# The second mixture of a two-mixture kernel on one core: counting of bids in groups of four tiles, search steps at finer points, a list chain on 43-wide arrays

## The chip, the cores and the metric

The program runs on one core of a Trainium2 chip. Its time is device microseconds of that core. It was timed in three runs (1503.53 to 1504.03 us, median 1503.86 us). Shares, chains and single durations come from one further execution with the profiler, which took 1500.03 us and whose span is 1498.2 us.

## The reference

An attention-like stage gives x (4608 tokens by 512). A first mixture of eight experts follows (top expert by a softmax router), then a second one, and this change is about the second:

```python
def _moe2_ref(x, w_gate, w1, w2):
    N, D = x.shape                       # 4608, 512
    E = w_gate.shape[1]                  # 8
    cap = N // E                         # 576
    flat = (x @ w_gate).flatten()
    order = np.argsort(-flat)
    assigned = -np.ones(N, dtype=np.int64)
    counts = np.zeros(E, dtype=np.int64)
    for idx in order:                    # best (token, expert) pair first
        tok, e = (int(idx) // E, int(idx) % E)
        if assigned[tok] >= 0 or counts[e] >= cap:
            continue
        assigned[tok] = e
        counts[e] += 1
    for e in range(E):
        mask = assigned == e
        h = np.maximum(x[mask] @ w1[e], 0.0)
        out[mask] = h @ w2[e]            # w1 512x1024, w2 1024x512
```

So every expert takes exactly 576 tokens, and which ones depends on the order in which experts fill up.

## The kernel before, in words

Three stages follow each other. Up to about 250 us runs the attention-like stage. Then come T1 = 43 tiles of 128 sorted rows through the first mixture ("stage one" below); after each tile VectorE computes the eight router scores of its rows from y (`scores`, L1198 to L1205). The rest is the second mixture: eight **phases**, one for each expert in the order in which the experts fill, each of T2 = 5 tiles of rows.

A tile is 48 **products** on TensorE (128x128 stationary, 512 columns, in fp32r). Every operand is split into a high and a low part, so each layer takes three passes (high by high, high by low weights, low by high weights): 12 products for each half of the first layer and 24 for the second. Beside them stand 4 transposes of the next tile's rows (L723) and 8 of h (L730). ScalarE makes the high parts and the copies, VectorE the low parts: `rows_low` (xT_lo, L1183), `hT_low` (hT_lo, L1189, two instructions a tile) and `weights_low` (w_lo, L1237, eight pieces of 1024 columns a phase). Weights come by SP's queue: eight pieces of 512 KB a phase, issued once the expert is known, with at most two on their way, and ScalarE waits until all eight have landed (L473, L936).

Which expert fills next, and with which rows, is found by **select** (L1263 to L1383) on VectorE with small steps on TensorE (`search`, L766 to L789). The scores are an array of 128 partitions x 43 tiles x 8 experts.

- *bids*: each row bids for its best open expert (`best`, `bid`, L1285 to L1292).
- *eight rounds* of a search for the threshold at which the first expert is full, 15 thresholds each: `cmp` on VectorE (128x645), a *count* on TensorE, `ind` on VectorE, a *spread* over partitions on TensorE, then `tn`, `n_i`, `low_i`, `thr_i`, which give the next 15 thresholds. The count is one matmul for each of the 43 tiles, with 128 bid columns as stationary side (8 of them in use) and 15 columns moving, plus one for the room left: 44 matmuls.
- *the list chain*: sums above and at the threshold, the expert (L1336, releases the weight load), ties, then the row numbers of the expert's rows: `ohb` (128x5504), `oha2`, `ra2`, one list step of 43 matmuls on TensorE (L787), `gat_i` and `sca_i` (L1376, releases the gathers of POOL), and last the scores of the filled expert and of the taken rows are masked (L1379 to L1383).

Each step is a pair: VectorE raises one semaphore (`ask`, L1275) and waits for TensorE's answer. Nineteen steps make a select. Of the order: a table gives each step a **point** among the products of the running phase. TensorE reaches a point, waits there for VectorE, does the step and goes on with the products; all its instructions stand in one order. The table of before has eight points a tile, and the next expert's select runs beside the running phase; its first eight steps (four rounds) run a phase earlier, from tile 3 on. VectorE puts its own duties for the products (`rows_low`, `hT_low`, `weights_low`) right behind its request of a step, before it waits for the answer (`beside_step`, L1250). Select 0, and the first four rounds of select 1, have no products beside them. VectorE runs selects 2 to 7 in a hardware loop of two selects an iteration.

Of the kernel before, what the change touches and what calls it, by code (L numbers as in the profile page):

```python
# [30 lines left out]
P = 128  # L31
# [28 lines left out]
def build(nc, q, k, v, g_norm, w_gate, w_og, w1, w2, w_gate2, w21, w22, out, debug=None):  # L60
# [4 lines left out]
    PT = 96  # L65
# [19 lines left out]
    STEPS = 2 * R + 3  # L85
    EARLY = 8
    gaps = [0] + [1, 2] * R + [4, 7]
    at, where = 0, []
    for n in range(STEPS):
        at += gaps[n]  # L90
        where.append(at)
    cycle = 8 * T2
    POINTS = sorted((x - where[EARLY]) % cycle for x in where)
    assert len(set(POINTS)) == STEPS and POINTS[0] == 0

    DUTIES = {n: [] for n in range(STEPS)}
    for g in range(T2):
        for kind, due, need in (("h", 8 * g, 8 * g + 5), ("x", 8 * g + 4, 8 * g + 8)):  # L100
            p = min([x for x in POINTS if x >= due], default=cycle)
            assert p <= need
            DUTIES[(POINTS.index(p) + EARLY) % STEPS if p < cycle else EARLY].append((kind, g))
    assert all(n != EARLY or ("x", T2 - 1) not in d for n, d in DUTIES.items())


    LOW_BESIDE = [EARLY - 4, EARLY - 3, EARLY - 2, EARLY - 1, EARLY + 4, EARLY + 5, EARLY + 6, EARLY + 7]
    PIECES = len(LOW_BESIDE)

    with ExitStack() as ctx:  # L110
# [24 lines left out]
        ones_h = sb("ones_h", [P, P], F16)  # L135
        before = sb("before", [P, P])
# [4 lines left out]
        segment = sb("segment", [PT, E, G1])  # L141
# [16 lines left out]
        onehot = sb("onehot", [PT, E, G1])  # L158
# [51 lines left out]
        s_wp = [sem(f"piece_loaded{i}") for i in range(2)]  # L210
# [5 lines left out]
        s_clear = sem("bids_cleared")  # L216
# [17 lines left out]
        s_sc = sem("scores_done")  # L234
        s_sel = sem("select_dve")
# [97 lines left out]
        bid = sb("bid", [P, T1, P], F16)  # L333
# [3 lines left out]
        cmp = sb("cmp", [P, T1, NTH], F16)  # L337
        a3 = sb("a3", [P, T1, E])
        b3 = sb("b3", [P, T1, E])
        taken = sb("taken", [P, T1, E])  # L340
        room_n = sb("room_n", [P, P], F16)
        ind = sb("ind", [P, NTH], F16)
        best = sb("best", [P, T1])
        m43 = sb("m43", [P, 4, T1])
        tn = sb("tn", [P, NTH])
        n_i = sb("n_i", [P, R], I32)
# [55 lines left out]
        def _(sp):  # L402
# [56 lines left out]
            def load_phase(kk, u):  # L459
# [27 lines left out]
        def _(pool):  # L487
# [84 lines left out]
            pool.memset(bid[:, :, :], 0.0).then_inc(s_clear, 1)  # L572
# [29 lines left out]
        def _(pe):  # L602
# [73 lines left out]
            def in_parts(ps, acts, w, cols, chunks, low_w, low_x, done, point):  # L676
# [3 lines left out]
                per = chunks * 3 // (2 if chunks == KC else 4)  # L680
                for i in range(3 * chunks):
# [9 lines left out]
                    if i % per == per - 1:  # L691
                        point(i // per)
# [71 lines left out]

            cps, aps = sel_ps

            def search(kk, n):
# [3 lines left out]
                if n < 2 * R and n % 2 == 0:  # L771
# [4 lines left out]
                elif n < 2 * R:  # L776

                    mm = pe.matmul(aps[:, 0:NTH], ones_h[:, :], ind[:, :], start=True, stop=True)
                elif n == 2 * R:

                    pe.matmul(cps[:, 0:2 * E], ones_h[:, :], sums_h[:, :, :], start=True, stop=True)
                    mm = pe.matmul(aps[:, 0:E], before_h[:, :], sums_h[:, 1, :], start=True, stop=True)
                elif n == 2 * R + 1:
# [8 lines left out]
            def searches(kk, i):  # L792


                if i in POINTS:
                    n = POINTS.index(i) + EARLY
                    ahead = kk + 1 if n < STEPS else kk + 2
                    if not (isinstance(kk, int) and ahead >= E):
                        search(ahead, n % STEPS)
# [631 lines left out]
```

## Time and profile before

| | us |
|---|---|
| median of three runs | 1503.86 |
| profiled execution | 1500.03 |
| its span | 1498.2 |
| last y of stage one made (ScalarE, L906) | 793.4 |
| first product of the second mixture (TensorE, L687) | 877.3 |
| TensorE busy in 787 to 890 us | 37.7 of 103 |
| TensorE busy in 890 to 1498 us | 580.8 of 608 |
| VectorE busy in 890 to 1498 us | 382.5 of 608 |

A row of the timeline gives start, duration, engine, line, instruction, and in brackets how long the engine was idle before it and who released it. "PE" is TensorE, "DVE" VectorE, "ACT" ScalarE, "POOL" GpSimd. Matmul ends are modelled, so the cost of a group on TensorE is best read as the distance from its start to the next start.

### The profile page before, as it was taken

Reading aid. Unit: us, or ns where it says so; the run is one execution under the profiler, and the core shown is the slowest. Engines: PE = TensorE matmul, PEld = TensorE weight load, DVE = VectorE, ACT = ScalarE, POOL = GpSimd, SP = SyncE. Lnnn points to the kernel's source line nnn. Section 1 sums busy time; section 2 is a strip of 40 time slices with the busy share of each in tenths; the row PEclk is TensorE's granted clock in tenths of the full one; section 3 lists DMA queues with packets and bytes.
Section 4 is the critical chain, followed back from the end, with each engine's and each line's share of the span. In section 5 each row is a group of like instructions: output and inputs, shape, how many; then the busy total and the mean of one; then the engine's idle time right before and its main releaser. Section 6 shows DMA issues by size and latency. Waiting matters only on the chain.

```text
span 1498.2 us, 26945 instructions
## 1 busy us (share of the span) xinstructions
PE 1315.6 (88%) x9724; PEld 1084.6 (72%) x9724; DVE 974.1 (65%) x2214; ACT 441.3 (29%) x784; POOL 397.5 (27%) x324
## 2 busy tenths in 40 slices
PE   5988718898999999999993169999999999999997
PEld 5877616786888888888882157878777777787885
DVE  1566793677567677776667768585758585767420
ACT  1655522122222222222220032423232323233431
POOL 1244426747616172480000001111111111111110
PEclk9989858999999999999996569999999999999999
DMA  9999128694514143241100304040404132222310
GB/s 218 253 271 289 57 45 297 220 352 154 156 43 155 42 157 106 89 146 49 43 22 15 124 18 148 30 152 30 145 30 132 50 117 65 82 93 84 104 32 18
DMA packets 71168, 173.48 MB, mean 116 GB/s; under 512 B 11624, under 2 KB 30136, under 8 KB 70400
## 3 DMA queue, kind: packets, MB, share of 16 engines
q1 hardware_dynamic: 46576, 108.61, 24.8%
q0 software_dynamic: 12368, 40.92, 8.6%
q10 hardware_dynamic: 12096, 22.19, 4.7%
q8 instruction: 87, 1.43, 0.4%
q14 instruction: 41, 0.34, 0.1%
HBM read 130.47 MB, written 41.23 MB: 115 GB/s over the span
## 4 chain that ended last, share of the span: by engine, by line
PE 67%; DVE 16%; DMA 6%; issue 5%; POOL 5%; ACT 1%; SPq 0%; DVEq 0%; POOLq 0%; ACTq 0%
PE bank L687 50%; PE bank L775 5%; PE bank L730 4%; POOL w_lo L524 3%; PE o_ps L648 2%; DMA xst<-x_rows,tok_i 2%; DMA x_sorted<-xst 1%; DMA v_sb<-in_v 1%; PE kv_ps L614 1%; POOL w_hi L522 1%; DMA w_sb<-in_moe_w 1%; PE bank L723 1%; PE bank L716 1%; DVE xrow L1052 1%; PE qt_ps L636 1%
## 5 line engine op out<-in xcount | busy, mean ns | idle before, releaser
L1202 DVE SCALAR_TENSOR_TENSOR bank<-bank,factor,wg2b 128x512 f32<-128x512 f32 x344 | 260.6, 758 | 10.8
L1189 DVE TENSOR_TENSOR hT_lo<-bank,hT_hi 128x512 fp32r<-128x512 f32 x166 | 107.0, 685 | 194.0 <-ACT hT_hi L932 185.0
L899 ACT ACTIVATE h<-bank 128x512 f32<-128x512 f32 x166 | 99.2, 598 | 356.8 <-PE bank L687 335.7
L687 PE MATMUL bank<-w_hi,xT_hi 128*128 (+1 forms) x664 | 193.1, 413 | 10.7 <-POOL w_lo L524 6.4
L687 PE MATMUL bank<-w_lo,xT_hi 128*128 (+1 forms) x664 | 190.6, 403 | 0.4 <-DVE w_lo L1237 0.4
L687 PE MATMUL bank<-w_hi,hT_hi 128*128 (+1 forms) x664 | 180.8, 411 | 6.2 <-DVE score L1205 3.3
L687 PE MATMUL bank<-w_hi,xT_lo 128*128 (+1 forms) x664 | 182.9, 397 | 0.0
L578 POOL DMA_INDIRECT xg<-y_rows,gat_i x40 | 41.6, 1040 | 502.3 <-DVE sca_i L1376 283.1
L687 PE MATMUL bank<-w_lo,hT_hi 128*128 (+1 forms) x664 | 173.4, 402 | 0.0
L687 PE MATMUL bank<-w_hi,hT_lo 128*128 (+1 forms) x664 | 171.0, 398 | 0.0
L687 PEld LDWEIGHTS bank<-w_hi,xT_lo 128*128 128x128 f32 x664 | 125.6, 189 | 30.5 <-issue 0.2
L687 PEld LDWEIGHTS bank<-w_lo,hT_hi 128*128 128x128 f32 x664 | 125.9, 191 | 29.4
L687 PEld LDWEIGHTS bank<-w_hi,hT_lo 128*128 128x128 f32 x664 | 124.2, 189 | 29.1
L687 PEld LDWEIGHTS bank<-w_hi,xT_hi 128*128 128x128 f32 x664 | 120.1, 193 | 33.8 <-issue 12.4
L687 PEld LDWEIGHTS bank<-w_lo,xT_hi 128*128 128x128 f32 x664 | 123.9, 191 | 28.0 <-DVE w_lo L1237 0.9
L687 PEld LDWEIGHTS bank<-w_hi,hT_hi 128*128 128x128 f32 x664 | 119.1, 191 | 28.2 <-issue 6.2
L524 POOL TENSOR_TENSOR w_lo<-w_sb,w_hi 128x1024 fp32r<-128x1024 f32 x56 | 134.3, 2398 | 4.5
L522 POOL CAST w_hi<-w_sb 128x1024 fp32r<-128x1024 f32 x56 | 58.3, 1041 | 183.0 <-DMA w_sb<-in_moe_w 183.0
L585 POOL DMA_INDIRECT out<-y,sca_i x40 | 44.8, 1120 | 230.2 <-ACT y L927 228.1
L1183 DVE TENSOR_TENSOR xT_lo<-bank,xT_hi 128x512 fp32r<-128x512 f32 x83 | 57.2, 690 | 72.6 <-ACT xT_hi L917 71.3
L932 ACT ACTIVATE hT_hi<-bank 128x512 fp32r<-128x512 f32 x166 | 90.8, 598 | 45.6 <-PE bank L730 33.7
L906 ACT ACTIVATE y<-bank,factor 128x512 f32<-128x512 f32 x43 | 29.5, 687 | 218.4 <-PE bank L687 193.5
(238 smaller groups left out, 1803.1 us busy)
## 6 DMA issues: line engine op xcount, KB each, us to landing
w_sb<-in_moe_w SPq DMA_DIRECT2D x112, 512.0 KB, 5.0
y_rows<-y ACTq DMA_DIRECT2D x43, 256.0 KB
x_sorted<-xst SPq DMA_DIRECT2D x41, 260.0 KB
xg<-x_sorted ACTq DMA_DIRECT2D x41, 260.0 KB
k_sb<-in_k SPq DMA_DIRECT2D x16, 576.0 KB, 15.5
v_sb<-in_v SPq DMA_DIRECT2D x16, 576.0 KB, 17.3
q_sb<-in_q SPq DMA_DIRECT2D x8, 1152.0 KB, 20.6
x_rows<-xrow POOLq DMA_DIRECT2D x16, 576.0 KB, 6.3
```

Source lines behind the costliest of these rows:

```text
L522: pool.tensor_copy(w_hi[:, 1 - e % 2, cols(i)], w_sb[:, e % 2, cols(i)]).then_inc(s_phi, 1)
L524: pool.tensor_tensor(w_lo[:, e % 2, cols(i)], w_sb[:, e % 2, cols(i)], w_hi[:, 1 - e % 2, cols(i)].bitcast(F32), ALU.subtract).then_inc(s_ ...
L578: pool.indirect_dma_start(out=xgs[w % 2][:, 0:DM], out_offset=None, in_=y_rows[:, :], in_offset=bass.IndirectOffsetOnAxis(ap=gat_i[:, w:w ...
L585: pool.indirect_dma_start(out=out[:, :], out_offset=bass.IndirectOffsetOnAxis(ap=sca_i[0:rows, w:w + 1], axis=0), in_=ys[w % 2][0:rows, :] ...
L687: mm = pe.matmul(ps, a[:, i % chunks, :], b[:, i % chunks, cols], start=(i == 0), stop=(i == 3 * chunks - 1))
L730: mm = pe.transpose(th_ps[half][:, i * P:(i + 1) * P], h[:, half * 4 + i:F:FC], ident[:, :])
L775: mm = pe.matmul(cps[:, 0:NTH], bid[:, g, :], cmp[:, g, :], start=False, stop=(g == T1 - 1))
L899: act.activation(h[:, half * HALF:(half + 1) * HALF], h_ps[half][:, :], ACT.Relu).then_inc(s_h, 1)
L932: act.activation(hT_hi[:, half * 4:(half + 1) * 4, :].rearrange("p a b -> p (a b)"), th_ps[half][:, :], ACT.Copy).then_inc(s_hT, 1)
L1183: dve.tensor_tensor(xT_lo[:, :, :].rearrange("p a b -> p (a b)"), tx_ps[:, :], xT_hi[:, :, :].rearrange("p a b -> p (a b)").bitcast(F32), ...
L1189: dve.tensor_tensor(hT_lo[:, half * 4:(half + 1) * 4, :].rearrange("p a b -> p (a b)"), th_ps[half][:, :], hT_hi[:, half * 4:(half + 1) * ...
L1202: ch.link(dve.scalar_tensor_tensor(out=prod_ps[:, :], in0=y1_ps[t % 2][:, :], scalar=factor[:, t:t + 1], in1=wg2b[:, e, :], op0=ALU.mult, ...
```

## The change

1. **Dense count.** `bid` shrinks from 43x128 to 43x8 columns. Four tiles go into one matmul: 32 stationary columns (4 tiles x 8 experts) and 60 moving ones (4 tiles x 15 thresholds). Eleven matmuls replace 43; the wanted numbers are the four diagonal blocks. A new step copies the 32x60 result to SBUF (`dense`, VectorE), and five small matmuls add the blocks and the room (TensorE). A round has three steps where it had two.
2. **List chain on 43-wide arrays.** Each row's bid is kept as one number (`code`), each row's owner too (`owner`), and ties and ranks are worked out on 128x43 arrays in place of 128x43x8 ones. Sums use the dense count; a step for ties is new. `ohb` is made in two halves with a duty between them.
3. **Points.** A point stands behind every second product: 24 a tile. The 29 steps of a select are laid out with ten points a round; it starts 13 points ahead of a phase, so five steps (one round and two steps of the next) run a phase earlier. A point of tile 4 holds the list step, and ten points on stands the first count of the select after it. The first phase has a table of its own, seven points a round, and select 1 runs wholly inside it.
4. **Duties.** The low parts of the next phase's first two weight pieces and of the last tile's h stand behind the list, ahead of the masking.
5. **Weights.** All eight pieces are issued at once, each with a semaphore of its own; ScalarE waits for a piece, not for all.
6. **Between the stages.** The last tile's router scores come from TensorE (4 transposes, a copy, 4 matmuls) in place of eight products on VectorE; the bids and first comparison of 40 of the 43 tiles are made two tiles earlier; the low parts of the first phase's first four pieces stand behind select 0's list.

Core of the diff:

```diff
+    GROUP = 4
+    SUMS, TOTALS, TIES, RANKS, LIST = range(3 * R, 3 * R + 5)
+    PER_TILE = 24
+    def timed(start, per_round, behind):
+        at = [start + per_round * r + 2 * i for r in range(R) for i in range(3)]
+        for gap in behind:
+            at.append(at[-1] + gap)
+        at += [at[LIST] - 8, at[LIST] + 3]
+        return at
+    WHERE = timed(-13, 10, (4, 3, 6, 5, 18))
+    FIRST = timed(13, 7, (3, 3, 5, 4, 17))
+        for kind, due, need in (("h", PER_TILE * g + 3, PER_TILE * g + 16), ("x", PER_TILE * g + 13, PER_TILE * g + 24)):
+    LOW_BESIDE = {AFTER_LIST: (0, 1), 1: (2,), 2: (3,), 7: (4,), 8: (5,), 10: (6,), 11: (7,)}
+    FIRST_LOW_BESIDE = {1: (4,), 2: (5,), 4: (6,), 5: (7,)}
...
-                    wait_pos(sp, s_wp[i % 2], (kk * (PIECES // 2) + i // 2) * 16)
                     sp.dma_start(w_sb[:, u, i * w_piece:(i + 1) * w_piece],
-                                 ).then_inc(s_wp[i % 2], 16)
+                                 ).then_inc(s_wp[i], 16)
...
+            pe.wait_ge(s_y, T1)
+            for c in range(KC):
+                mm = pe.transpose(tx_ps[:, c * P:(c + 1) * P], ys[(T1 - 1) % 2][:, c * P:(c + 1) * P], ident[:, :])
+            for c in range(KC):
+                mm = pe.matmul(th_ps[0][:, 0:E], h[:, c * P:(c + 1) * P], wg2_sb[:, c, :], start=(c == 0), stop=(c == KC - 1))
...
-                    pe.matmul(cps[:, 0:NTH], room_n[:, :], ones_h[:, 0:NTH], start=True, stop=False)
-                    for g in range(T1):
-                        mm = pe.matmul(cps[:, 0:NTH], bid[:, g, :], cmp[:, g, :], start=False, stop=(g == T1 - 1))
+                    for g in range(0, T1, GROUP):
+                        some = min(GROUP, T1 - g)
+                        mm = pe.matmul(dps[0:some * E, 0:some * NTH], bid[:, g:g + some, :].rearrange("p g e -> p (g e)"),
+                                       cmp[:, g:g + some, :].rearrange("p g n -> p (g n)"), start=(g == 0), stop=(g + GROUP >= T1))
+                    pe.matmul(cps[0:E, 0:NTH], room_n[:, :], ones_h[0:1, 0:NTH], start=True, stop=False)
+                    for g in range(GROUP):
+                        mm = pe.matmul(cps[0:E, 0:NTH], ident_h[:, g * E:(g + 1) * E], dense[:, g * NTH:(g + 1) * NTH],
+                                       start=False, stop=(g == GROUP - 1))
...
-                    if i % per == per - 1:
-                        point(i // per)
+                    if i % 2 == 1:
+                        point(i // 2)
...
-                act.wait_ge(s_wl, (kk + 2) * 32)
                 for i in pieces:
+                    act.wait_ge(s_wp[i], (kk + 1) * 16)
...
+                if n == AFTER_LIST:
+                    for i in LOW_BESIDE[n]:
+                        weights_low(kk, u, i)
...
+                    ask(dve.tensor_copy(dense[:, :], dps[0:GROUP * E, :]))
-                link(dve.tensor_tensor(b3[:, :, :], b3[:, :, :], over_g(es), ALU.mult))
-                link(dve.tensor_reduce(m43[:, 0, :], b3[:, :, :], AX, ALU.add))
-                link(dve.tensor_tensor(b3[:, :, :], b3[:, :, :], over_e(m43[:, 1, :]), ALU.mult))
-                link(dve.tensor_tensor(a3[:, :, :], a3[:, :, :], b3[:, :, :], ALU.add))
-                link(dve.tensor_tensor(taken[:, :, :], taken[:, :, :], a3[:, :, :], ALU.add))
+                link(dve.scalar_tensor_tensor(out=tied, in0=rank, scalar=spare, in1=tied, op0=ALU.is_le, op1=ALU.mult))
+                link(dve.tensor_tensor(chosen, gteq[:, :, 0], tied, ALU.add))
+                    link(dve.tensor_tensor(tied, chosen, code[:, :], ALU.mult))
+                    link(dve.tensor_tensor(owner[:, :], owner[:, :], tied, ALU.add))
+                link(dve.tensor_scalar(mine, owner[:, :], expert, None, ALU.is_equal))
...
+                    if gs.start == 0:
+                        beside_step(kk, u, HALF_LIST)
...
+                beside_step(kk, u, AFTER_LIST)
```

The order on TensorE between the list step of one select (matmuls bank<-ra,ohb) and the first count of the next (bank<-cmp,bid), inside the loop over phases. Before:

```order
L787 MATMUL bank<-ra,ohb 128x20 x42
...
L730 MATMUL bank<-ident,h 128x128 x3
...
L687 MATMUL bank<-w_hi,xT_lo 128x512 x3
L721 ISA
L723 MATMUL bank<-ident,xg 128x128 [waits y_rows_gathered0]
L723 MATMUL bank<-ident,xg 128x128 x3
L687 MATMUL bank<-w_hi,hT_hi 128x512 [waits y_ready,hT_copied]
L687 MATMUL bank<-w_hi,hT_hi 128x512 x5
L770 ISA
L773 MATMUL bank<-ones_h,room_n 128x15 [waits select_dve]
L775 MATMUL bank<-cmp,bid 128x15 x43
```

Now:

```order
L838 MATMUL bank<-ra,ohb 128x20 x42
L710 MATMUL bank<-w_lo,xT_hi 128x512 x4
L710 MATMUL bank<-w_hi,xT_lo 128x512 [waits xT_low]
L710 MATMUL bank<-w_hi,xT_lo 128x512 x3
L710 MATMUL bank<-w_hi,xT_hi 128x512 x4
L710 MATMUL bank<-w_lo,xT_hi 128x512 x4
L710 MATMUL bank<-w_hi,xT_lo 128x512 [waits xT_low]
L710 MATMUL bank<-w_hi,xT_lo 128x512 x3
L804 ISA
L811 MATMUL bank<-cmp,bid 32x60 [waits select_dve]
L811 MATMUL bank<-cmp,bid 32x60 x9
L811 MATMUL bank<-cmp,bid 24x45
```

Before, 30 products, 12 transposes stood between the two (8 of h, all 24 products of the first layer, 4 transposes of rows, 6 products of the second layer); now 20 products and no transpose.

The order on VectorE from the list's last instruction (sca_i) to the first comparison of the next select. Before:

```order
L1376 SCALAR_TENSOR_TENSOR sca_i<-lst 128x5
L1379 TENSOR_REDUCE m<-a 128x43
L49 REGISTER_ALU
L1380 TENSOR_SCALAR m<-m 128x43 [waits dve_chain]
L1381 TENSOR_SCALAR e<-e 128x8
...
L1299 TENSOR_TENSOR cmp<-best,thr 128x645 [waits dve_chain]
L1188 ISA
L1189 TENSOR_TENSOR hT_lo<-bank,hT_hi 128x512 [waits hT_copied]
```

Now:

```order
L1463 SCALAR_TENSOR_TENSOR sca_i<-lst 128x5
L1319 ISA
L1321 TENSOR_TENSOR w_lo<-w_sb,w_hi 128x1024 [waits weights_high]
L1319 REGISTER_ALU
L1321 TENSOR_TENSOR w_lo<-w_sb,w_hi 128x1024 [waits weights_high]
L1245 ISA
L1246 TENSOR_TENSOR hT_lo<-bank,hT_hi 128x512 [waits hT_copied]
L1245 REGISTER_ALU
L1246 TENSOR_TENSOR hT_lo<-bank,hT_hi 128x512 [waits hT_copied]
L1467 SCALAR_TENSOR_TENSOR room<-e 128x8
L1468 TENSOR_SCALAR m<-m 128x43
```

Two pieces of w_lo and one tile's hT_lo now stand between the list and the masking; the chain from masking to comparison is otherwise the same, without one reduction.

The order on TensorE in tile 0 of the first phase, behind its 24 first-layer products (there is no second layer of an earlier tile yet). Now:

```order
L746 MATMUL bank<-ident,xg 128x128 x3
L811 MATMUL bank<-cmp,bid 32x60 [waits select_dve]
L811 MATMUL bank<-cmp,bid 32x60 x9
L811 MATMUL bank<-cmp,bid 24x45
L815 MATMUL bank<-ones_h,room_n 8x15 [waits select_dve]
L817 MATMUL bank<-dense,ident_h 8x15 x4
L821 MATMUL bank<-ind,ones_h 128x15 [waits select_dve]
L811 MATMUL bank<-cmp,bid 32x60 [waits select_dve]
L811 MATMUL bank<-cmp,bid 32x60 x9
L811 MATMUL bank<-cmp,bid 24x45
L815 MATMUL bank<-ones_h,room_n 8x15 [waits select_dve]
L817 MATMUL bank<-dense,ident_h 8x15 x4
```

Five steps of select 1 stand there in a row with no product between them.

## Rows read from the trace of the kernel before

**Rows 1.** Windows: span, us, busy (count) PE PEld DVE ACT POOL, PEclk, DMA share, GB/s

```profile
890.00:1498.00 608.00, 580.76 (x4940) 469.05 (x4940) 382.48 (x872) 183.15 (x292) 82.25 (x76) 0.99 0.26 81
```

**Rows 2.** Timeline (start, us, engine, line, instruction, shape, count), TensorE, two tiles without steps

```profile
1405.71 1.05 PE L730 MATMUL bank<-ident,h 128*128 128x128 f32 x8
...
1416.40 2.03 PE L687 MATMUL bank<-w_hi,hT_lo 128*128 128x512 f32 x8
1418.27 1.05 PE L730 MATMUL bank<-ident,h 128*128 128x128 f32 x8
```

**Rows 3.** Timeline, TensorE, a count and a spread between products

```profile
1192.20 0.18 PE L773 MATMUL bank<-ones_h,room_n 128*128 128x15 f16 x1
...
1193.33 0.71 PE L687 MATMUL bank<-w_lo,xT_hi 128*128 128x512 f32 x2
...
1194.81 0.18 PE L778 MATMUL bank<-ind,ones_h 128*128 128x15 f16 x1
...
1195.86 1.09 PE L687 MATMUL bank<-w_lo,xT_hi 128*128 128x512 f32 x4
```

**Rows 4.** Timeline, TensorE, the transposes of h that close tiles

```profile
893.23 1.95 PE L730 MATMUL bank<-ident,h 128*128 128x128 f32 x8
...
954.60 1.05 PE L730 MATMUL bank<-ident,h 128*128 128x128 f32 x8
...
1031.52 1.05 PE L730 MATMUL bank<-ident,h 128*128 128x128 f32 x8
```

**Rows 5.** Timeline, from the list step to the next select's first count

```profile
999.88 1.24 PE L787 MATMUL bank<-ra,ohb 128*128 128x20 f16 x43
...
1006.92 0.83 DVE L1299 TENSOR_TENSOR cmp<-best,thr 128x645 f16<-128x645 f32 x1
...
1242.28 0.16 DVE L1285 TENSOR_SCALAR room_n<-room 1x8 f16<-1x8 f32 x1 [3.37 <-issue]
...
1246.31 0.18 PE L773 MATMUL bank<-ones_h,room_n 128*128 128x15 f16 x1 [1.57 <-DVE cmp L1299]
```

**Rows 6.** Groups by shape (count, busy us, mean ns, idle and releaser), VectorE, phases

```profile
L1237 DVE TENSOR_TENSOR w_lo<-w_sb,w_hi 128x1024 fp32r<-128x1024 f32 x59 | 71.5, 1219 | 0.0
L1189 DVE TENSOR_TENSOR hT_lo<-bank,hT_hi 128x512 fp32r<-128x512 f32 x80 | 51.5, 684 | 45.8 <-ACT hT_hi L932 45.6 <-DVE score L1383 0.2
...
L1379 DVE TENSOR_REDUCE m<-a 128x43 f32<-128x344 f32 x7 | 3.5, 504 | 0.0
```

**Rows 7.** Windows around two stops of TensorE, columns as in rows 1

```profile
886.00:898.00 12.00, 8.16 (x116) 7.17 (x114) 8.33 (x18) 4.17 (x6) 0.95 (x1) 0.72 0.08 23
1090.00:1098.00 8.00, 8.00 (x73) 6.27 (x72) 2.32 (x10) 1.15 (x2) 0.99 (x1) 0.79 0.00 0
```

**Rows 8.** Timeline, from the last y to the first phase; then DMA issues

```profile
793.44 0.69 ACT L906 ACTIVATE y<-bank,factor 128x512 f32<-128x512 f32 x1 [6.05 <-PE bank L687]
...
807.58 0.20 PE L773 MATMUL bank<-ones_h,room_n 128*128 128x15 f16 x1 [14.18 <-DVE cmp L1299]
...
839.58 0.14 DVE L1336 TENSOR_SCALAR expert_i<-sc 1x1 int32<-1x1 f32 x1
...
856.06 0.17 DVE L1376 SCALAR_TENSOR_TENSOR sca_i<-lst 128x5 int32<-128x5 f32 x1
...
861.19 5.79 ACT L939 ACTIVATE w_hi<-w_sb 128x1024 fp32r<-128x1024 f32 x6 [67.06 <-SPq L473]
...
877.28 2.05 PE L687 MATMUL bank<-w_hi,xT_hi 128*128 128x512 f32 x4 [0.78 <-ACT xT_hi L917]
...
891.57 0.20 PE L773 MATMUL bank<-ones_h,room_n 128*128 128x15 f16 x1 [3.57 <-DVE cmp L1299]
...
xg<-y_rows,gat_i POOLq DMA_INDIRECT x40, 3.4
```

**Rows 9.** Timeline, TensorE's rank step and VectorE's last part of a list

```profile
1224.64 0.18 PE L784 MATMUL bank<-mtot_h,before_h 128*128 128x1 f16 x1 [1.00 <-DVE mtot_h L1356]
...
1233.22 1.05 DVE L1369 TENSOR_TENSOR ra<-oha,payload 128x860 f16<-128x860 f16 x1
```

More of the change, by code:

```diff
@@ L82, in build @@
     STAGED = 8
[L85 to L98, printed above, removed]
-    for g in range(T2):
[L100 to L103, printed above, removed]
@@ new lines, in build @@
+    WHERE = timed(-13, 10, (4, 3, 6, 5, 18))
+    FIRST = timed(13, 7, (3, 3, 5, 4, 17))
+    EARLY = sum(x < 0 for x in WHERE)
+    POINTS = {x % cycle: n for n, x in enumerate(WHERE[:STEPS])}
+    FIRST_POINTS = {x: n for n, x in enumerate(FIRST[:STEPS])}
+    assert len(POINTS) == STEPS and len(FIRST_POINTS) == STEPS and AFTER_LIST == len(WHERE) - 1
+    assert max(FIRST) < WHERE[0] + cycle
+    DUTIES = {n: [] for n in range(len(WHERE))}
+    FIRST_DUTIES = {n: [] for n in range(len(WHERE))}
@@ L336, in build @@
         ohb = sb("ohb", [P, T1, P], F16)
[L337 to L344, printed above, removed]
-        tn = sb("tn", [P, NTH])
+        sb("rest_of_router", [P, 560])
+        oha2 = sb("oha2", [P, T1, T2], F16)
+        ra2 = sb("ra2", [P, T1, T2, 4], F16)
+        tn = sb("tn", [P, NTH])
+        gteq = sb("gteq", [P, T1, 2], F16)
+        blocks = sb("blocks", [GROUP * E, GROUP, 2])
+        sums = sb("sums", [GROUP * E, 2])
+        spread = sb("spread", [GROUP * E, 2, E], F16)
+        e8 = sb("e8", [P, 4, E])
         n_i = sb("n_i", [P, R], I32)
@@ L770, in search @@
                 pe.wait_ge(s_sel, kk * STEPS + (n + 1))
-                if n < 2 * R and n % 2 == 0:
-                    pe.matmul(cps[:, 0:NTH], room_n[:, :], ones_h[:, 0:NTH], start=True, stop=False)
-                    for g in range(T1):
-                        mm = pe.matmul(cps[:, 0:NTH], bid[:, g, :], cmp[:, g, :], start=False, stop=(g == T1 - 1))
[L776 to L783, printed above, removed]
+                if not isinstance(kk, int):
+                    alone(pe)
@@ L792, in searches @@
             def searches(kk, i):
+                first = isinstance(kk, int) and kk == 0
+                if first and i in FIRST_POINTS:
+                    search(1, FIRST_POINTS[i])
                 if i in POINTS:
[L796 to L799, printed above, removed]
+                    n = POINTS[i]
+                    ahead = kk + 1 if n >= EARLY else kk + 2
+                    if not (first and n >= EARLY) and not (isinstance(kk, int) and ahead >= E):
+                        search(ahead, n)
             def phase(j, u):
@@ L826, in _ @@
                 search(0, n)
-            for n in range(EARLY):
-                search(1, n)
             y_rows_in(0, 0, 0)
@@ L1209, in _ @@
             first_low(range(PIECES // 2, PIECES))
-            for t in range(T1 + 2):
+            for t in range(T1 + 1):
                 if t > 2:
@@ L1331, in select @@
-                link(dve.tensor_tensor(w8, at, left, ALU.is_ge))
+                tied, rank, chosen, mine, cum = (m43[:, i, :] for i in (0, 2, 3, 4, 5))
+                left, w8, es, t8 = (e8[:, i, :] for i in range(4))
+                expert, spare, ties_before, mine_before = (sc1[:, i:i + 1] for i in range(4))
+                link(dve.tensor_scalar(gteq[:, :, 0], best[:, :], top, None, ALU.is_gt))
+                ask(dve.tensor_scalar(gteq[:, :, 1], best[:, :], top, None, ALU.is_equal))
```

297 lines of the change are left out of this document (182 added, 115 removed).

## The prediction

> **What bounds the kernel now.** First the windows: over the phases TensorE is busy 581 of 608 us and VectorE 382 [rows 1], so TensorE's own stream sets the pace; every step's matmuls and every wait at a point lengthen it. Then TensorE's timeline. Two tiles without steps lie 12.56 us apart; eight products take 1.87 us, 0.234 each, so 48 are 11.2 us and 12 transposes with their switches 1.3 [rows 2]. A count (44 matmuls) pushes the next product 1.13 us back, 26 ns a matmul. A spread (one matmul) with four products takes 1.05 us, four products 0.93: 0.12, of which some 0.09 is the switch; so a count is 1.2 [rows 3]. A phase takes 76.9 us [rows 4]: 62.8 for products, 8 x 1.32 = 10.6 for rounds, 1.4 for the list chain's steps, and some 2 of waits. Third, the rows ahead of the first phase: from the last y (793.4) to the first product (877.3) TensorE only serves select [rows 8]. This stretch of 84 us is the only other place of weight.
>
> **Counting (parts 1 and 3).** A round becomes 11 + 5 + 1 = 17 matmuls in three places. At 26 ns and 0.07 to 0.09 for each place: 0.35 + 0.20 + 0.12 = 0.67 us against 1.32, so 0.65 saved. The unknown is the cost of 60 moving columns. Products give 0.234 us for 512, so 27 ns for 60, no more than the row's 26 ns for 15; that I take. The other bound is a whole product, 0.234 each: 11 x 0.21 = 2.3 us more a count, 129 us over 56 rounds; a 128-column transpose is nearer, about 0.1 us each (eight before 12.56 - 11.2 us ran out), 0.8 more a count, 45 us. Below, a matmul can't come under the 26 ns of the row. The Trainium skill (TensorE: Matmul & The Clock Gate, Back-to-back issue gap) gives a floor of about 25 ns for any width from 1 to 64 columns; by it eleven matmuls are 0.28 us, the same sum. The list chain grows: sums 0.35, three steps at 0.12, list 1.17 make 1.9 against 1.4, 0.5 lost. A phase saves 8 x 0.65 - 0.5 = 4.7 us.
>
> **The new wait behind the list (parts 3 and 4).** This is the step on which I lean most. Before, from the list step to the end of the next select's first comparison VectorE takes 1006.92 + 0.83 - 999.88 = 7.87 us, and TensorE's stream between the two is so long (30 products, 12 transposes) that it waits only where VectorE's loop turns (3.37 us of "issue"): 1.57 us [rows 5]. Now the stream between is 20 products: 20 x 0.234 + 1.17 for the list itself = 5.85 us. VectorE has lost one reduction (0.54) and gained two w_lo (2 x 1.22) and two hT_lo (1.29) [rows 6]: 7.87 - 0.54 + 2.44 + 1.29 + 0.07 = 11.1 us. So TensorE stops 5.3 us each time, in phases 0 to 5, and 3.4 more in the two where the loop turns, as VectorE has no cover left there. Queued behind that count are the transposes of the next rows and the 24 products of the second layer; VectorE itself waits for nobody. Both ends: with w_lo and hT_lo at no cost it is 1.6 us; if w_lo also waits for ScalarE, another us.
>
> Each stop has a second price. After the 3.57 us stop [rows 8] the window shows a granted clock of 0.72 over 12 us, thus 6.7 us at 1.2 GHz of 2.4; behind the other turn of VectorE's loop, near 1090, it is 0.79 over 8 us, 3.4 us at half [rows 7]. Half speed costs half of the busy part of it. With the shorter one that is 1.7 us for each stop; I take 1.7, since a part of a longer stretch falls into the stop. The Trainium skill says the same of such gaps (same page, HAM oscillation): each stop is paid again by a stretch of slow matmuls. By it the dense count can be lost to the clock; the trace agrees with the direction, and the size above is the rows'.
>
> **Smaller waits.** Rank step to the end of `ra2` took 1233.22 + 1.05 - 1224.64 = 9.63 us [rows 9]. With xT_lo (0.69) and the split of ohb (0.1) in between it is 10.4; the stream of 36 products and 12 transposes there is 9.8: 0.65 of wait. Ties to ranks is a chain of eleven small instructions of about 0.25 with their links, 3.05 us, against ten products, 2.4: 0.65. Inside the rounds (low parts in the gaps of two points) 0.4. A steady phase before had 1.7 of such waits, 1.0 of it at the rank step [rows 9].
>
> Steady phase: 76.9 - 4.7 - 1.7 + (5.3 + 1.7 + 1.7) = 79.2, **2.3 slower**, for phases 1, 3, 5. In 2 and 4 before had a wait and a slow stretch already (1.6 to 2.1 and 1.7), now 3.4 to 4.0 more: 2.0 slower each. Phase 6 has no such stop and more rounds of its own: 0.4 faster. Phase 7 is as before. Sum 6.9 + 4.0 - 0.4 = **+10.5**.
>
> **The start (parts 5 and 6).** First count before: 807.6. Now y is there at 794.1; transposes, copy, four narrow matmuls and the min make 796.2 (the scores of the tile ahead of it end before that); bids for three tiles and their comparison 1.6: 797.9, 9.7 us earlier. A round stays near 3.4 us, as 11 matmuls at the slow clock and one more handover weigh as much as 44. The sums without 344-wide arrays give 1.7, so the expert is known 11.4 us earlier (839.6 to 828.2), and the list ends 13.4 earlier (856.1 to 842.7) as its 344-wide links are gone. Before, four rounds of select 1 stood before the first product; now they don't. What is late next: w_hi, whose copies began only when all pieces were in (861.2, 21.6 us after the expert). Now the sixth piece is in at 828.2 + 21.6 x 6/8 = 844.4 and w_hi at 845.4 (5.79 us were six copies); gathers 842.9 + some 4.5 (median landing 3.4, more beside weights) = 847.5; four w_lo behind the list 847.6. Then transposes at half clock and xT_hi: first product at 849.3, **28 us earlier** than 877.3 [rows 8]. Bounds: 31 if pieces come at the best rate, 13.4 if only the list counts.
>
> **The first phase (part 3).** Its first tile took 893.2 - 877.3 = 15.9 us, the other four to 954.6 [rows 4]: 61.4. Now five steps stand in a row there without a product, with w_hi 6 and 7 on ScalarE ahead of xT_hi, xT_lo and two w_lo on VectorE between them: 8.2 for the products, then some 9.7 of handovers: 17.9, 2 more. The other four: 50.2 of products and transposes, 4.0 for six rounds, 1.9 list chain, 1.2 for select 2's first steps, 2.4 for the slow clock after the row of steps, 3.6 at rounds (seven points are 3.3 us of products for a chain of 3.1 plus duties), 2.3 at ties and ranks (hT_lo stands between), 5.7 + 1.7 at the stop behind the list: 73 less 1 by which the same count overshoots before. **+12.5** with the first tile.
>
> **Sum.** -28 + 12.5 + 10.5 = -5 us. The profiled execution would take 1495, and as the median stands 3.8 above it, I predict **1499**. The rest (stage one, the last phase, the tail) is hidden or unchanged: VectorE's early bids (3.9 us, the chain from 1242.28 to the count) lie ahead of the last tile's hT_lo, for which VectorE waits on ScalarE anyway; without that cover they cost up to 3.9.
>
> **Rivals.** (A) *Slower: the stops are dearer.* If every one of the six behaves like the one at 891.6, with 6.7 us of half clock in busy time, each costs 3.4 and not 1.7: +10, 1509. For it: that stop of 3.57 us is nearer to 5.3 than the 2 us one. Against: the slow stretch there overlaps the stop. It decides from 2.5 us a stop. (B) *The stop is not there or short*, because TensorE's stream between is longer than I count or VectorE takes its duties elsewhere: 6 x 7.0 + 3.4 + 3.4 less, about 1455. Against it stands the plain order of both engines. Half of it, 1477, is easier. (C) *The start is held* by weights or gathers while eight pieces share the queues: only 13.4 of 28, 1513. (D) *Wide matmuls in the count cost like transposes*: 1540.
>
> **Chances.** Forecast (own range 1492 to 1505) 0.50; A 0.20; B 0.08, half of B 0.10; C 0.07; D 0.05. Two kernels within 0.2%, 3 us, can't be told apart here. Faster by over that: 0.35 of the forecast and B, 0.53. Same: 0.16. Slower: 0.31. The range that leaves out B and D is 1478 to 1513.
>
> **What would show it.** In the profile of the changed kernel: the first count of each select waits 5 us on cmp (about 9 in two phases), in six phases; PEclk dips behind each; a count of 11 matmuls pushes products 0.3 us; first product near 849; phases of about 79 us against 76.9; a first phase near 90. The forecast is wrong if those waits are under 2 us or phases shorter than 75.

## The result and the profile after

The changed kernel is slower. Its median is 1533.04 us over four runs (1527.43 to 1540.84), the kernel before measured beside it has 1503.69: a ratio of 1.0195, with a 95% interval of 1.0158 to 1.0232. Forecast was 1499, so the time lies some 34 us above it and outside the range. The profiled execution took 1531.16 us, its span is 1529.4.

Windows of both kernels, each from the first product of the second mixture to the end (span, us, busy and count of PE PEld DVE ACT POOL, PEclk, DMA share, GB/s). After:

```profile
848.00:1529.00 681.00, 614.38 (x3747) 459.64 (x3747) 373.70 (x941) 188.18 (x298) 84.55 (x78) 0.95 0.21 73
```

Before, the line for 877 to 1498:

```profile
877.00:1498.00 621.00, 591.47 (x5058) 477.43 (x5058) 386.52 (x882) 186.86 (x298) 83.92 (x78) 0.98 0.25 80
```

TensorE does 1300 matmuls fewer, waits more, and is *busy* 23 us longer. Timeline of TensorE after, the rows that answer to [rows 5, 8]: the start, then the first count of each select (in brackets the idle time before it and who ended it).

```profile
848.60 2.05 PE L710 MATMUL bank<-w_hi,xT_hi 128*128 128x512 f32 x4 [0.78 <-ACT xT_hi L970]
...
930.97 0.72 PE L811 MATMUL bank<-cmp,bid 128*32 128x60 f16 x11 [5.38 <-DVE cmp L1277]
...
1015.26 0.72 PE L811 MATMUL bank<-cmp,bid 128*32 128x60 f16 x11 [5.04 <-DVE cmp L1277]
...
1102.15 0.70 PE L811 MATMUL bank<-cmp,bid 128*32 128x60 f16 x11 [8.52 <-DVE cmp L1277]
...
1186.36 0.70 PE L811 MATMUL bank<-cmp,bid 128*32 128x60 f16 x11 [5.14 <-DVE cmp L1277]
...
1280.23 0.70 PE L811 MATMUL bank<-cmp,bid 128*32 128x60 f16 x11 [8.45 <-DVE cmp L1277]
...
1364.19 0.70 PE L811 MATMUL bank<-cmp,bid 128*32 128x60 f16 x11 [5.13 <-DVE cmp L1277]
```

The start at 848.6 (849.3 forecast) and the six stops (5.3 and 8.7 forecast) are there, to a few tenths. What is not as forecast stands inside the rounds. One round among products, TensorE, which answers to [rows 3]:

```profile
1128.70 1.18 PE L710 MATMUL bank<-w_hi,xT_hi 128*128 128x512 f32 x4
1129.71 1.10 PE L710 MATMUL bank<-w_lo,xT_hi 128*128 128x512 f32 x4
1130.74 0.48 PE L811 MATMUL bank<-cmp,bid 128*32 128x60 f16 x11
1131.15 1.19 PE L710 MATMUL bank<-w_hi,xT_lo 128*128 128x512 f32 x4
1132.27 0.17 PE L815 MATMUL bank<-ones_h,room_n 1*8 1x15 f16 x1
1132.30 0.24 PE L817 MATMUL bank<-dense,ident_h 32*8 32x15 f16 x4
1132.47 1.21 PE L710 MATMUL bank<-w_hi,xT_hi 128*128 128x512 f32 x4
1133.61 0.18 PE L821 MATMUL bank<-ind,ones_h 8*128 8x15 f16 x1
1133.72 1.20 PE L710 MATMUL bank<-w_lo,xT_hi 128*128 128x512 f32 x4
1134.75 1.09 PE L710 MATMUL bank<-w_hi,xT_lo 128*128 128x512 f32 x4
1135.68 0.51 PE L746 MATMUL bank<-ident,xg 128*128 128x128 f32 x3
```

From 1128.70 to 1135.68 are 24 products (5.61 us at 0.234) and three steps, and it takes 1.37 us more than the products alone. Of this 0.08 is no step's: behind the closing transposes the first four products take 1.01 us (1128.70 to 1129.71), and so they do in a tile of the kernel before that has no step:

```profile
1406.52 1.17 PE L687 MATMUL bank<-w_hi,xT_hi 128*128 128x512 f32 x4
1407.53 1.09 PE L687 MATMUL bank<-w_lo,xT_hi 128*128 128x512 f32 x4
1408.46 1.10 PE L687 MATMUL bank<-w_hi,xT_lo 128*128 128x512 f32 x4
```

That leaves 1.29 us for the three steps here. Over all steps at full clock behind 935 us (medians of some 30 of each kind, from the product ahead to the second one behind, less two products) a count costs 0.61 us, the block sums 0.39 and a spread 0.31: 1.31 a round. The forecast had 0.67, and the two steps of before take 1.34 in the same way (1.21 and 0.13). Nobody waits here. The extra time stands at the borders: four products between two steps take 1.12 to 1.14 us from start to start, and 0.93 with no step near. The weight load row of each step (PEld) shows a gap ahead of it, 0.35 to 0.37 us, where the steps of before in [rows 3] have 0.27:

```profile
1132.27 0.08 PEld L815 LDWEIGHTS bank<-ones_h,room_n 1*8 1x8 f16 x1 [0.35 <-issue]
...
1133.60 0.09 PEld L821 LDWEIGHTS bank<-ind,ones_h 8*128 8x128 f16 x1 [0.37 <-issue]
```

The column 1*8 or 8*128 is the stationary side. A product's is 128*128; no step of the kernel before has another ([rows 3] show 128*128 for the spread too), and all three steps of a new round have.

The closing transposes of the phases, as in [rows 4]:

```profile
941.39 1.16 PE L753 MATMUL bank<-ident,h 128*128 128x128 f32 x8
...
1024.73 1.16 PE L753 MATMUL bank<-ident,h 128*128 128x128 f32 x8
...
1112.33 1.16 PE L753 MATMUL bank<-ident,h 128*128 128x128 f32 x8
```

The first steady phase takes 83.3 us (79.2 forecast, 76.9 before), the next, with VectorE's loop turn, 87.6. Phases 3 to 5 take 86.2, 91.6 (with the loop turn) and 84.5. And the granted clock around the stop of 1186 is 0.57 over twelve microseconds, mostly its lower level of 1.2 GHz, where [rows 7] have 0.72 and 0.79:

```profile
1184.00:1196.00 12.00, 9.64 (x38) 7.02 (x39) 7.13 (x17) 0.60 (x1) 0.97 (x1) 0.57 0.11 38
```

Counted from windows of 1 us each, as busy time times what the clock lacks of 1, the half clock costs 24.4 us after and 8.0 before, in the windows above. Waits of TensorE sum to 57.7 us after and 21.0 before. From the first product to the end it is 680.8 us against 620.9, 59.9 more: 36.7 of waits, 16.4 of clock, and 6.8 of longer work, where 28 less had been expected of the steps (4.7 a phase in six phases). The start gives 28.7 back.

### The profile page after: what moved, and what is told of

It is laid out like the page before. It is cut to its first block, busy times and chain, and to the rows that moved or that the text cites. A ratio compares the mean times of both kernels' runs of the same rounds, so it can differ in the third digit from the quotient of the medians.

```text
span 1529.4 us, 23677 instructions
## 1 busy us (share of the span) xinstructions
PE 1331.3 (87%) x8032; PEld 1058.7 (69%) x8032; DVE 942.4 (62%) x2229; ACT 443.9 (29%) x785; POOL 394.3 (26%) x323
## 3 DMA queue, kind: packets, MB, share of 16 engines
q8 instruction: 74, 1.21, 0.3%
## 4 chain that ended last, share of the span: by engine, by line
PE 65%; DVE 17%; DMA 6%; issue 5%; POOL 4%; ACT 1%; SPq 1%; DVEq 0%; POOLq 0%; ACTq 0%
PE bank L710 49%; PE bank L753 4%; DVE ohb L1452 3%; PE o_ps L672 2%; POOL w_lo L548 2%; PE bank L811 2%; DMA xst<-x_rows,tok_i 2%; PE bank L746 1%; PE kv_ps L638 1%; DMA x_sorted<-xst 1%; DMA v_sb<-in_v 1%; POOL w_hi L546 1%; PE bank L739 1%; PE qt_ps L660 1%; DVE xrow L1107 1%
## 5 line engine op out<-in xcount | busy, mean ns | idle before, releaser
L1259 DVE SCALAR_TENSOR_TENSOR bank<-bank,factor,wg2b 128x512 f32<-128x512 f32 x336 | 254.5, 758 | 10.4
L602 POOL DMA_INDIRECT xg<-y_rows,gat_i x40 | 48.7, 1217 | 574.2 <-DVE sca_i L1463 404.4
L710 PE MATMUL bank<-w_hi,hT_hi 128*128 (+1 forms) x664 | 190.8, 426 | 5.9 <-DVE score L1262 3.3
L710 PE MATMUL bank<-w_hi,xT_lo 128*128 (+1 forms) x664 | 186.8, 403 | 0.0
L710 PE MATMUL bank<-w_lo,hT_hi 128*128 (+1 forms) x664 | 177.4, 404 | 0.0
L710 PE MATMUL bank<-w_hi,hT_lo 128*128 (+1 forms) x664 | 174.6, 400 | 0.0
L710 PEld LDWEIGHTS bank<-w_hi,xT_hi 128*128 128x128 f32 x664 | 120.8, 194 | 38.0 <-issue 15.5
L710 PEld LDWEIGHTS bank<-w_hi,hT_hi 128*128 128x128 f32 x664 | 124.1, 200 | 29.0 <-issue 5.2
L980 ACT ACTIVATE y<-bank 128x512 f32<-128x512 f32 x40 | 23.9, 597 | 233.5 <-PE bank L710 233.5
```

The source lines that it names most:

```text
L602: pool.indirect_dma_start(out=xgs[w % 2][:, 0:DM], out_offset=None, in_=y_rows[:, :], in_offset=bass.IndirectOffsetOnAxis(ap=gat_i[:, w:w ...
L710: mm = pe.matmul(ps, a[:, i % chunks, :], b[:, i % chunks, cols], start=(i == 0), stop=(i == 3 * chunks - 1))
L1259: ch.link(dve.scalar_tensor_tensor(out=prod_ps[:, :], in0=y1_ps[t % 2][:, :], scalar=factor[:, t:t + 1], in1=wg2b[:, e, :], op0=ALU.mult, ...
```

## The experiments

Each was timed in three to five rounds beside the kernel before; three chips served (e1 to e4, e5 to e7, e8 to e10), so kernels are compared by their ratios to the kernel before. T1 is the theory that a stationary side smaller than the array costs time beside full ones; the second theory is that the stops come from what stands between the list and the next first count, and are a price of their own. Since stage one ended up to 11 us later in some profiles (last y at 790 to 801), I also give the time from the first product to the end of the profiled span; the changed kernel has 680.8.

**e1_full: all stationary sides full.**

```diff
-    mm = pe.matmul(dps[0:some * E, 0:some * NTH], bid[:, g:g + some, :]...
+    mm = pe.matmul(dps[:, 0:some * NTH], bid[:, g:g + 16, :]...
-    pe.matmul(cps[0:E, 0:NTH], room_n[:, :], ones_h[0:1, 0:NTH], ...
+    pe.matmul(cps[:, 0:NTH], room_n[:, :], ones_h[:, 0:NTH], ...      # room_n, ident_h: 128x128, zeros around
-    mm = pe.matmul(aps[:, 0:NTH], ones_h[0:E, :], ind[:, :], ...
+    mm = pe.matmul(aps[:, 0:NTH], ones_h[:, :], ind[:, :], ...        # ind, spread: 128 rows
```

> The changed kernel with every search step's stationary side 128 rows by 128 columns, padded with zeros (the number of matmuls, of steps, of moving columns, of waits and their places is the same). T1, the cost of a step comes from matmuls whose stationary side is smaller than the array: they do not overlap with the full products around them. Then a round costs 0.35 + 0.1 for eleven, five and one matmuls at 26 ns plus three switches of 0.09, about 0.72 us in place of 1.37, for 56 rounds 0.65 x 56 = 36 us less: about 1497 us, and 24 products and a round take 6.3 us and not 6.98. T2, the cost lies in having three places instead of two (registers, semaphore waits, change of operand type at each): no change, about 1533. T3, it lies in the 60 moving columns of the count: no change either, and the excess stays with the count alone.

Measured: 1497.31 us, ratio to before 0.9977 (0.9957 to 0.9997); 647.0 us from the first product, 33.8 less. The round, TensorE's timeline:

```profile
1111.76 1.18 PE L710 MATMUL bank<-w_hi,xT_hi 128*128 128x512 f32 x4
1112.77 1.08 PE L710 MATMUL bank<-w_lo,xT_hi 128*128 128x512 f32 x4
1113.70 0.48 PE L811 MATMUL bank<-cmp,bid 128*128 128x60 f16 x11
1114.02 1.16 PE L710 MATMUL bank<-w_hi,xT_lo 128*128 128x512 f32 x4
1115.03 0.18 PE L815 MATMUL bank<-ones_h,room_n 128*128 128x15 f16 x1
1115.07 0.25 PE L817 MATMUL bank<-dense,ident_h 128*128 128x15 f16 x4
1115.17 1.19 PE L710 MATMUL bank<-w_hi,xT_hi 128*128 128x512 f32 x4
1116.20 0.18 PE L821 MATMUL bank<-ind,ones_h 128*128 128x15 f16 x1
1116.24 1.18 PE L710 MATMUL bank<-w_lo,xT_hi 128*128 128x512 f32 x4
1117.26 1.10 PE L710 MATMUL bank<-w_hi,xT_lo 128*128 128x512 f32 x4
1118.19 0.64 PE L746 MATMUL bank<-ident,xg 128*128 128x128 f32 x4
```

The same 24 products and three steps take 6.43 us in place of 6.98, so 0.82 above the products where it was 1.37 (the 0.08 behind the transposes is in both). By the medians, taken as above, a count costs 0.41 us, the block sums 0.23 and a spread 0.12: 0.76 a round in place of 1.31, and 0.09 above the forecast's 0.67. The count still moves 60 columns and pushes the next product back by 0.32 (from 1113.70 to 1114.02), 0.41 before; so neither the width of the moving side nor the three places were dear. T2 and T3 fall. The padding is not zeros everywhere: `bid[:, g:g + 16, :]` fills the count's other 96 columns with the bids of the next twelve tiles (zeros past the last), and their sums are left unused. The waits stayed (59.3 us).

**e2_rows8: the reverse, in the kernel before.**

```diff
-    mm = pe.matmul(aps[:, 0:NTH], ones_h[:, :], ind[:, :], start=True, stop=True)
+    mm = pe.matmul(aps[:, 0:NTH], ones_h[0:E, :], ind[0:E, :], start=True, stop=True)
```

> The kernel before, with one edit: the spread matmul takes only the 8 rows that carry numbers as its contraction side, in place of 128. T1 (partial stationary side is dear beside full products): 0.1 us ahead of and 0.1 us behind each of the 56 spreads that stand among products, +10 us, about 1514. T2 or T3: nothing, 1504 within 2.

Measured: 1512.28 us, 1.0080 (1.0051 to 1.0109), about 12 us slower, by making one matmul a round smaller. The spread and its neighbours, TensorE; in [rows 3] the spread with four products is 1.05:

```profile
1179.97 0.63 PE L687 MATMUL bank<-w_lo,xT_hi 128*128 128x512 f32 x2
1180.54 0.18 PE L778 MATMUL bank<-ind,ones_h 8*128 8x15 f16 x1
1180.64 0.74 PE L687 MATMUL bank<-w_lo,xT_hi 128*128 128x512 f32 x2
1181.22 1.09 PE L687 MATMUL bank<-w_hi,xT_lo 128*128 128x512 f32 x4
```

Here it is 1.25 (1179.97 to 1181.22): 0.10 more ahead of it, 0.10 behind. By the medians a spread costs 0.31 us here and 0.13 in the kernel before. The forecast counts 56 spreads, but in this kernel four of them stand ahead of the first product: 52 at 0.18 are 9.5 us, inside what the times allow (8 to 16). The output is 128 by 15 in both, so here it is missing rows, of both operands, that are dear, and no column.

**e5_count_full: only the counts and sums full.**

```diff
     count and sums as in e1_full; room, blocks, spread and totals as in the changed kernel
```

> The changed kernel with only the counts and the sums padded to 128 stationary columns; room, block sums, spread and totals keep their small sides. Theory T1b, each partial matmul group between full products has its own price of about 0.2 us: of the 36 us that padding everything gives, the counts' third goes, 63 groups x 0.2 = 12 us, about 1520. Rival, the price is paid once a round (whichever step is still partial): no change, 1531. Rival, the counts carry all of it, as they have eleven partial matmuls and the others one to five: about 1500.

Measured: 1516.55 us, 1.0119 (1.0084 to 1.0154). The counts' part is 1.0195 - 1.0119, 11 us; the other steps' 1.0119 - 0.9977, 21 us, for twice as many places. That is 0.18 us for each of 63 counts and sums and the same for each of 119 other places; each of the two differences is uncertain by 6 to 8 us. The trace is sharper: here a count costs 0.41 us, as in e1, and the block sums 0.39 and a spread 0.30, as in the changed kernel. So small sides cost 0.20 us at a count (eleven matmuls), 0.16 at the block sums (five) and 0.19 at a spread (one): the price is per place, whether one matmul stands there or eleven. In the counts it is columns alone that are missing (32 of 128). Within a place it is not paid: in the changed kernel the block sums change from 1*8 to 32*8 in 0.03 us (1132.27, 1132.30).

**e3_gap24: the list 24 points ahead.**

```diff
-    WHERE = timed(-13, 10, (4, 3, 6, 5, 18))
+    WHERE = timed(-13, 8, (4, 3, 6, 5, 18))
```

> The changed kernel with one number of its table changed: rounds at 8 points in place of 10, so that the list step stands 24 points ahead of the first count of the next select and not 10; the first phase keeps its own table. TensorE's stream between is then 48 products and 12 transposes, 12.6 us, against VectorE's chain of 11.1 (14.5 where its loop turns). Theory: the stops at the first count in phases 1 to 5 go from 32.3 us to about 4, the slow stretches behind them with them (16 us of lost busy time in those phases to about 4); inside the rounds nothing new waits, as rounds of 7 points in the first phase did not; -28 - 12 = -40, about 1493. Rival, the stops only move: the eight points of a round are too short beside the duties and the sums, and 2 us of waits a phase come back in the rounds: about 1505. Rival, VectorE is itself the bound of a phase: the phase stays above 84 us and the time above 1520.

Measured: 1553.66 us, 1.0345 (1.0314 to 1.0375): some 20 us slower than the changed kernel, a miss. The stops at the first count did shrink (40.5 us of waits on cmp to 16.7), but 17.3 on xT_lo and 15.7 more on ind came, 69.2 in all, and the clock's loss rose to 32.6. Behind a list step, all engines:

```profile
1178.07 1.23 PE L838 MATMUL bank<-ra,ohb 128*128 128x20 f16 x43 [1.14 <-DVE ra L1458]
...
1186.97 2.01 ACT L992 ACTIVATE w_hi<-w_sb 128x1024 fp32r<-128x1024 f32 x2
1188.07 2.36 DVE L1321 TENSOR_TENSOR w_lo<-w_sb,w_hi 128x1024 fp32r<-128x1024 f32 x2 [7.93 <-ACT w_hi L992]
1190.35 0.68 DVE L1240 TENSOR_TENSOR xT_lo<-bank,xT_hi 128x512 fp32r<-128x512 f32 x1
1191.09 1.87 PE L710 MATMUL bank<-w_hi,xT_lo 128*128 128x512 f32 x4 [2.86 <-DVE xT_lo L1240]
```

The list moved, and with it w_lo, which stands behind the list by the table; but ScalarE makes these w_hi at the end of the phase's fourth tile, which did not move. VectorE waits 7.93 us for them, and xT_lo stands behind. The time lies where the last rival had it, but these rows show VectorE waiting for ScalarE and not busy with work of its own. So the gap may be right and the duties in it wrong, which e6 tests.

**e4_full_gap24: both edits.**

```diff
     stationary sides as in e1_full, WHERE as in e3_gap24
```

> Both edits: stationary sides padded to 128 by 128, and 24 points between the list and the next first count. If the step cost (T1) and the stops are separate prices, the gains add: -36 and -40 of 1533, about 1457. If the cheaper steps only uncover VectorE (shorter stream, same chains), part of the first comes back as waits, about 1470. If T1 is wrong, it equals the one with the gap alone.

Measured: 1533.04 us, 1.0223 (1.0189 to 1.0256). Padding is again worth 1.0345 - 1.0223, 18 us here, less than beside the old table: waits rose to 74.3, so part of it only uncovers VectorE. Both forecasts, 1457 and 1470, rest on the 40 us of e3, which did not come.

**e6_tab: the table laid out anew.** The changed kernel, small sides and all, with this table (`timed` takes the rounds' lengths one by one; HALF_LIST 14 points ahead of the list, AFTER_LIST 5 behind):

```diff
-    WHERE = timed(-13, 10, (4, 3, 6, 5, 18))
+    WHERE = timed(-8, (9, 9, 9, 7, 8, 9, 7), (4, 2, 4, 6, 20), -14, 5)
-    LOW_BESIDE = {AFTER_LIST: (0, 1), 1: (2,), 2: (3,), 7: (4,), 8: (5,), 10: (6,), 11: (7,)}
+    LOW_BESIDE = {0: (0,), 1: (1,), 2: (2,), 3: (3,), 6: (4,), 7: (5,), 9: (6,), 12: (7,), AFTER_LIST: ()}
```

> The changed kernel with another table and nothing else: rounds of 7 to 9 points, the list step 22 points ahead of the next first count, select starting 8 points ahead of a phase, no weight piece behind the list: its eight low parts stand beside the steps of the first four rounds, where the high parts are made by then. What went wrong with 24 points was where the duties landed (two weight pieces behind the list had to wait for their high parts, and the next rows' low part stood behind them; two duties stood ahead of one ind). Theory: with these off the chain the stops go altogether; waits of TensorE 57.7 to about 18 (the first phase keeps 12), busy time lost to half clock 24 to about 10: -40 - 14, about 1479. Rival, VectorE is the bound whatever the order: waits stay above 50, and the time above 1520.

Measured: 1480.44 us, 0.9876 (0.9840 to 0.9912): 3.2% below the changed kernel, 48 us. From the first product 627.6 us, 53.2 less. Waits 57.7 to 20.1, clock loss 24.4 to 5.0. Behind a list step of it, all engines:

```profile
1144.94 1.25 PE L838 MATMUL bank<-ra,ohb 128*128 128x20 f16 x43
...
1146.85 0.17 DVE L1463 SCALAR_TENSOR_TENSOR sca_i<-lst 128x5 f32 x1
...
1151.57 0.83 DVE L1277 TENSOR_TENSOR cmp<-best,thr 128x645 f16<-128x645 f32 x1
...
1157.84 0.48 PE L811 MATMUL bank<-cmp,bid 128*32 128x60 f16 x11
```

VectorE is ready at 1152.40, 7.5 us behind the start of the list step, as nothing stands between the list and the masking any more; TensorE comes at 1157.84, without a stop. The edit moves the gap and the duties together, and no run moves the duties alone (e3 moves the gap alone), so what each of the two is worth is not shown. Over 400 us of steady phases, changed kernel first, then this one:

```profile
940.00:1340.00 400.00, 365.46 (x2300) 269.54 (x2296) 229.46 (x600) 112.69 (x177) 49.63 (x45) 0.95 0.21 72
```

```profile
940.00:1340.00 400.00, 390.98 (x2541) 288.96 (x2539) 260.70 (x674) 124.52 (x197) 57.10 (x52) 1.00 0.25 86
```

**e7_full_tab, e9_full_tab2, e10_full_tab3: padded sides with three tables.** e7 has that of e6. The other two:

```diff
+    WHERE = timed(-7, (15, 8, 9, 9, 9, 7, 9), (5, 2, 2, 8, 19), -13, 6)    # e9
+    LOW_BESIDE = {1: (0,), 2: (1, 2, 3), 4: (4,), 7: (5,), 9: (6,), 12: (7,), AFTER_LIST: ()}
+    WHERE = timed(-8, (9, 9, 9, 8, 9, 9, 9), (3, 3, 4, 8, 19), -12, 2)     # e10
+    LOW_BESIDE = {0: (0,), 1: (1,), 2: (2,), 3: (3,), 6: (4,), 7: (5,), 10: (6,), 13: (7,), AFTER_LIST: ()}
```

> Both cures together: all stationary sides 128 by 128, and the table without stops. If step cost and stops are two separate prices, both are saved: 1533 - 36 - 54 = about 1443. If the shorter stream of TensorE uncovers VectorE's chain, a third of it comes back as waits: about 1460. A phase then takes 71 to 73 us, against 76.9 in the kernel before.

> Padded sides, with a table laid out for the shorter stream: the first count of a select stands 28 points behind the list step (22 in the table before it) and takes only the next rows' low part (the low part of h stands beside the list step itself), rounds 1 to 4 get 15, 8, 9 and 9 points, the weight pieces stand one step later. In the profile of the first padded table the phases lost 4.8 us each: 1.0 at dense, 0.8 at the third count, 0.6 at w_lo. Theory: those waits were duties one or two steps too early, and go: about 1450, phases of 71 us, and 73 where VectorE's loop turns. Rival, with 71 us of products a phase VectorE's own chain with its duties is as long as the phase, so that waits only change their place: 1459 as before.

> Padded sides, with the table of the earlier padded kernel changed only a little: one point more in three of the rounds and two more between ties and ranks, the list step 17 points ahead of the next first count. Theory: the waits of 0.8 us at the third count go, dense keeps its 1.0: about 1455. Rival: VectorE's turn of the loop (3.4 us) shows again as a stop in two phases, as the list stands closer: 1459 or more.

> The changed kernel as it is, beside the two that follow, so that they and it share a chip and the runs of the kernel before: 1533 within 8, and 1.8 to 2.1% above the kernel before.

Measured: e7 1459.07 us, 0.9716 (0.9682 to 0.9749); e9 **1451.84, 0.9667 (0.9633 to 0.9702)**; e10 1457.18, 0.9705 (0.9669 to 0.9741); the changed kernel again 1533.82, 1.0201 (1.0160 to 1.0242). With the stops gone, padding is worth 0.9876 - 0.9716, 24 us and not 33: the shorter stream uncovers VectorE (its dense waits 9.1 us and cmp 8.5 in e7, from 7.7 and 5.5 in e6; all waits 27.0, from 20.1). The expectation for e9 says that its first count stands 28 points behind the list step; by its table it is 14, against 22 in e7, and the rounds and duties differ too. Its waits on dense fell from 9.1 to 3.5 us, as forecast. In e10 they did not fall (10.2 on dense, 9.5 on cmp), and waits of 0.5 us on cmp are new where VectorE's loop turns: its theory failed, and its rival is borne out in part. The intervals of e7, e9 and e10 overlap; from the first product e9 takes 595.0 us, e7 604.9 and e10 605.8. The phases of e9 come 72.0 us apart, 74.1 and 75.8 where VectorE's loop turns, and its steady stretch runs at full clock:

```profile
940.00:1340.00 400.00, 391.07 (x2709) 298.81 (x2708) 273.54 (x721) 128.39 (x205) 59.52 (x53) 1.00 0.25 87
```

e9 beats both kernels: 3.3% below the one before, 5.2% below the changed one.

## Why the prediction was wrong, step by step

- **The step that failed: "26 ns a matmul and 0.07 to 0.09 for each place", 0.67 us a round.** It measured 1.31. The small stationary sides stood in the sum at nothing, and they cost 0.55 a round (e1): 0.16 to 0.20 a place (e2, e5), 33 us over the kernel, almost all of the 34 by which the time was missed. The rest is 0.09 a round, as a full place costs 0.09 to 0.13 us beside its 26 ns a matmul, where I had 0.08. The row that I took the switch from, the spread of [rows 3], had a full side; the diff said `ones_h[0:E, :]` and `dps[0:some * E`, and I priced the number of matmuls and the moving columns and never this. Of the count's 60 moving columns I was right. Rival D's 1540 comes nearest to the measured time, but by luck: its reason, dear wide matmuls, is refuted by e1. The Trainium skill (TensorEngine Tiling (Array Packing), Key Properties) says that a change of tiling mode drains TensorE. The gaps fit that, 0.35 to 0.37 us ahead of a small side's weight load and 0.27 ahead of a padded one, but no run here shows which mode the engine was in.
- **The stops behind the list**: right. 37.7 us at six first counts, forecast 38.6; e6 removes them by the table alone, of which it changes the gap and the duties together.
- **The clock behind the stops**: direction right, size too small. I had about 9 us more than before; it was 16.4. With full sides, and the same stops, it is 10.9 (18.9 against 8.0). In the changed kernel phases 1 to 5 lost 1.6, 2.5, 4.8, 3.9 and 2.9 us, nearer to rival A's 3.4 a stop; with full sides 2.0, 1.8, 1.4, 3.6 and 1.6, nearer to my 1.7. Why equal stops lose so unequally is open.
- **The start**: right, 28.7 us earlier (28 forecast), with the last y at 793.4 before and 793.2 after.
- **The first phase**: +12.5 forecast, +15.5 measured (848.60 to 941.39), and +11.7 with full sides.
- **Smaller waits**: at rank and list step 0.5 and 0.67 (0.65 each forecast); inside the rounds none, where I had 0.4. A wait of 2.64 us on w_hi where TensorE's own loop turns, in one phase, I had not seen. What causes it is open.
- **The sum** for a steady phase was 79.2. Phases 1, 3 and 5 took 83.3, 86.2 and 84.5 us, and with full sides 79.1 each; the whole kernel with full sides takes 1497 against the 1499 forecast. That agreement is partly luck, as the dearer place and the clock are offset by waits that didn't come; but it says that one term carried the miss. A slip that changes nothing: rival B's terms add up to 48.8 less than 1499, 1450 and not 1455.
- **The signs**: none of what I had named as showing the forecast wrong, waits under 2 us or phases under 75, came about. The one sign for a round, a count that pushes products 0.3 us, measured 0.41 and was the one that failed.

## What to carry to other kernels

Before cutting a small matmul's rows or columns to those in use, look at what its neighbours have: here, between products with full 128x128 stationary sides, a small one cost 0.2 us a place, and filling it up to 128x128 cost nothing that these runs show. A table of duties is tied to the other engines' times: moving one step moves its duties past the producers of their inputs, so move them apart. And a stop costs more than its wait: taking out 38 us of waits in e6 gave 53.

## What was not expected of the hardware

- A step whose stationary side has 8 of 128 rows (e2), or 32 of 128 columns (e5), costs about 0.2 us more between fp32r products than one with all 128 by 128: 0.1 ahead, 0.1 behind. Sides between 32 and 128 were not run.
- Eleven matmuls with 60 moving columns and a full stationary side push the next product back by 0.32 us, and with the slower start of the products behind them they cost 0.41 (e1).
- The changed kernel spreads more from run to run (1527 to 1541) than the first three runs of before (1503.5 to 1504.0); in the experiments the kernel before itself spread from 1495.6 to 1508.9. Why is open.
